# First expert tile: its x loaded early and its last rows added by matmuls; table and rank work moved behind it

## What is computed

```python
# 1 attention: full attention on inputs averaged over 4 tokens, repeated 4 times,
#   plus attention in a band |i-j| < 4 at full resolution
out_up = np.repeat(sm_attn(q_d, k_d, v_d), 4, axis=2)
scores = np.where(np.abs(pos[:, None] - pos[None, :]) < 4, scale * q @ k.T, -1e9)
x = out_up + softmax(scores) @ v                     # -> (2304, 512)
# 2 experts: 8 experts, each token goes to the best one only
logits = norm(x) @ norm(expert_emb).T / tau
expert_idx = np.argmax(logits, axis=1)
gate_w = softmax(logits)[arange, expert_idx]
out[mask] = gate_w[mask, None] * (relu(x[mask] @ w1[e]) @ w2[e])   # w1 512x1024, w2 1024x512
# 3 a dense layer: h = x @ w_in (512x2048); out = max(0.01*h, h) @ w_out
```

## Time and profile before

| | us |
|---|---|
| median of 3 runs | 922.05 |
| lowest and highest of them | 920.63, 927.44 |
| the profiled execution, its own time | 920.19 |
| span of the profile | 918.4 |
| TensorE busy in the span | 876.5 |
| VectorE, ScalarE, GpSimd busy | 537.9, 508.7, 177.3 |
| mean granted TensorE clock | 0.993 of full speed |

### The profile page before, as it was taken

How to read it: one execution, slowest core, us unless ns; L and a number is a source line. 1 busy time by engine, 2 the same in 40 slices (tenths; PEclk the granted TensorE clock), 3 DMA queues, 4 the chain that set the end, 5 groups by cost and what they waited for, 6 DMA issues and landing times.

```text
span 918.4 us, 17213 instructions
## 1 busy us (share of the span) xinstructions
PE 876.5 (95%) x5880; PEld 737.2 (80%) x5880; DVE 537.9 (59%) x797; ACT 508.7 (55%) x912; POOL 177.3 (19%) x259
## 2 busy tenths in 40 slices
PE   8898986899999999999998999999999999999997
PEld 4787765577777777787787998998898898898896
DVE  5677763789987888889987554224223223223222
ACT  3677775588887888888887443223223223223222
POOL 8666763014311101120001001101101101100000
PEclk9999998999999999999999999999999999999999
DMA  7586566418457627271101000100100100100000
GB/s 222 162 238 204 179 206 222 166 46 254 167 179 281 226 91 298 77 290 36 47 23 58 1 1 25 45 1 23 46 0 19 49 0 15 54 0 12 24 1 34
DMA packets 44844, 92.39 MB, mean 101 GB/s; under 512 B 4616, under 2 KB 23928, under 8 KB 40704
## 3 DMA queue, kind: packets, MB, share of 16 engines
q1 hardware_dynamic: 34928, 44.26, 15.9%
q0 software_dynamic: 9872, 47.53, 13.9%
HBM read 72.97 MB, written 18.81 MB: 100 GB/s over the span
## 4 chain that ended last, share of the span: by engine, by line
PE 80%; DVE 7%; issue 5%; ACT 5%; POOL 2%; another core or an unknown queue 0%; DVEq 0%; ACTq 0%; DMA 0%; SPq 0%; POOLq 0%
PE banks L872 69%; PE banks L807 2%; PE banks L904 2%; ACT ehi L1122 1%; DVE elo L1467 1%; PE banks L785 1%; DVE xTlo L1472 1%; PE banks L712 1%; PE banks L749 1%; PE banks L720 1%; PE banks L923 1%; ACT pdin L1025 1%; PE banks L761 1%; PE banks L779 1%; PE banks L879 1%
## 5 line engine op out<-in xcount | busy, mean ns | idle before, releaser
L1467 DVE TENSOR_TENSOR elo<-wslot,ehi 128x1024 fp32r<-128x1024 f32 x196 | 237.6, 1224 | 37.2 <-ACT ehi L1122 27.6
L1122 ACT ACTIVATE ehi<-wslot 128x1024 fp32r x196 | 204.9, 1059 | 44.6 <-PE banks L872 36.9
L1541 DVE SCALAR_TENSOR_TENSOR fg<-fraw 128x384 f32<-128x384 f32 x96 | 53.5, 557 | 212.5 <-ACT fraw L1209 203.0
L1209 ACT ACTIVATE fraw<-banks 128x384 f32<-128x384 f32 x96 | 47.2, 492 | 227.9 <-PE banks L872 226.9
L872 PE MATMUL banks<-zhi,winhi 128*128 (+1 forms) x384 | 130.5, 340 | 0.2 <-issue 0.2
L872 PE MATMUL banks<-zhi,winlo 128*128 (+1 forms) x384 | 129.4, 337 | 0.0
L872 PE MATMUL banks<-zlo,winhi 128*128 (+1 forms) x384 | 129.0, 336 | 0.0
L872 PE MATMUL banks<-wouthi,fhi 128*128 128x512 f32 x288 | 113.1, 393 | 3.4 <-DVE flo L1546 2.5
L872 PE MATMUL banks<-wouthi,flo 128*128 128x512 f32 x288 | 113.9, 395 | 0.0
L872 PE MATMUL banks<-woutlo,fhi 128*128 128x512 f32 x288 | 113.7, 395 | 0.0
L872 PE MATMUL banks<-ehi,xThi 128*128 128x512 f32 x200 | 83.1, 416 | 7.1 <-DVE xTlo L1472 7.1
(11 more groups left out here) (217 smaller groups left out, 1435.7 us busy)
## 6 DMA issues: line engine op xcount, KB each, us to landing
wslot<-in_w POOLq DMA_DIRECT2D x24, 1024.0 KB
wslot<-in_w SPq DMA_DIRECT2D x8, 1024.0 KB
xr<-xs SPq DMA_DIRECT2D x25, 272.0 KB
ys<-y_sb SPq DMA_DIRECT2D x25, 256.0 KB
qb<-in_qT SPq DMA_DIRECT2D x16, 288.0 KB, 4.0
kb<-in_kT SPq DMA_DIRECT2D x16, 288.0 KB, 4.9
vq<-in_vtok SPq DMA_DIRECT2D x32, 144.0 KB
vwin<-in_vtok SPq DMA_DIRECT2D x16, 245.0 KB
```

The costliest lines, as they stand in the source:

```text
L1122: act.activation(ehi[:, ring_at(k), :], wslot[:, chunk_cols(offs[dt], matrix, half, c)], ACT.Copy).then_inc(s_ehi, 1)
L1209: act.activation(fraw[:, f % 2, :], banks[:, f % 2, 0:TB], ACT.Copy).then_inc(s_fhev, 1)
L1467: dve.tensor_tensor(elo[:, ring_at(k), :], wslot[:, chunk_cols(offs[dt], matrix, half, c)], ehi[:, ring_at(k), :].bitcast(F32), ALU.subtra ...
L1541: dve.scalar_tensor_tensor(out=fg[:, f % 2, :], in0=fraw[:, f % 2, :], scalar=0.01, in1=fraw[:, f % 2, :], op0=ALU.mult, op1=ALU.max).then ...
```

## The change

Seven things, in the order of the program:

1. GpSimd clears `xs[0:128]` and the dummy rows at step 6 instead of the dummy rows alone ahead of step 0. Batch 0's scatter waits for that.
2. SyncE loads rows 0 to 127 of `xs` as soon as batches 0 to 2 are scattered, and GpSimd scatters batch 3 only after this load. The quarters of expert 1's weights are spread: the first goes ahead of the last `load_v`, the last behind tile 1's x.
3. VectorE makes `hot`, one 128x128 matrix of zeros and ones for each of batch 3's five tiles: a one where a token's `pos` is a row of tile 0. TensorE's `gather_x` multiplies batch 3's x by them and adds the early-loaded rows, which are turned by a multiplication with the identity, in the same PSUM bank: tile 0's x, turned. The `warm` matmuls change (12 and 5 instead of 4, 16, 12 and 16).
4. Tile 0's first weight chunks are rounded without the tables (expert 0 is always in the first half). The tables (`tables()`, with fewer steps) come after tile 0's x on VectorE; one step is folded into others (`skip`).
5. The gates' logits, the sorted ranks (two parts) and the gates' sums go behind tiles 1, 2, 3 and 4 on VectorE, the `Exp` on ScalarE into tile 2.
6. The loops over expert tiles are written out on TensorE, ScalarE, VectorE and SyncE; clearing of an expert's tail rows goes with the loads of x, one per tile.
7. GpSimd waits, for each expert from 2 on, until the first two quarters of its weights have landed before it issues the other two; the gates' scatters move from experts 2, 3, 4 to 5, 6, 7, behind the signal `s_w`.

```diff
@@ SyncE
+            load_quarter(1, 0)
             sp.wait_ge(s_o6, NPAIR - 3)
             load_v(NPAIR - 1)
-            for n in range(4):
-                if n:
-                    sp.wait_ge(s_wfirst[1], 16 * n)
-                load_quarter(1, n)
+            sp.wait_ge(s_wfirst[1], 16)
+            load_quarter(1, 1)
+            sp.wait_ge(s_zrow, 32)
+            for b in range(B - 1):
+                sp.wait_ge(s_scat[b], 16 * (TILES[b][1] - TILES[b][0]))
+            sp.wait_ge(s_o6, NPAIR)
+            sp.dma_start(xr[:, 0, :], xs[0:P, :]).then_inc(s_xl[0], 16)
+            sp.wait_ge(s_wfirst[1], 32)
+            load_quarter(1, 2)
...
             zero_rows(0)
-            sp.wait_ge(s_zero, 16)
-            for b in range(B):
-                sp.wait_ge(s_scat[b], 16 * (TILES[b][1] - TILES[b][0]))
-            sp.wait_ge(s_zrow, 16)
+            zero_rows(1)
+            sp.wait_ge(s_scat[B - 1], 16 * (TILES[B - 1][1] - TILES[B - 1][0]))
             sp.wait_ge(s_tab, 1)
-            sp.dma_start(xr[:, 0, :], xs[0:P, :]).then_inc(s_xl[0], 16)
-            for e in range(1, E):
-                zero_rows(e)
-            sp.wait_ge(s_zero, 16 * E)
-            load_x(1, 1)
...
+            for t in range(1, NT):
+                if t >= 2:
+                    sp.wait_ge(s_mx, t - 1)
+                if t < E:
+                    sp.wait_ge(s_zero, 16 * (t + 1))
+                load_x(t, t % 2)
+                if t + 1 < E:
+                    zero_rows(t + 1)
+                if t == 1:
+                    load_quarter(1, 3)
+                if t >= 3:
+                    store_y(t - 3)
@@ GpSimd
             for s in range(NSTEP):
+                if s == 6:
+                    gp.wait_ge(s_ready, 1)
+                    for at0 in (0, DUMMY):
+                        gp.dma_start(xs[at0:at0 + P, :], zrow[:]).then_inc(s_zrow, 16)
...
             indices(B - 1)
+            gp.wait_ge(s_xl[0], 16)
             scatter(B - 1, 0, MT)
...
                 for n in range(4):
+                    if n == 2:
+                        gp.wait_ge(s_wl[e % SLOTS], 64 * (e // SLOTS - 1) + 32)
@@ TensorE
-            warm(4, 3)
+            warm(12, 3)
             ranks(B - 1, NPAIR - 1)
-            warm(16, 3)
-            pe.wait_ge(s_tab, 1)
-            warm(12, 3)
-            pe.wait_ge(s_scat[B - 1], 16 * MT)
-            warm(16, 3)
+            warm(5, 3)
...
+            def gather_x():
+                pe.wait_ge(s_xr, 2 * NPAIR)
+                for j in range(MT):
+                    if j in (0, 2):
+                        pe.wait_ge(s_hot, 1 if j == 0 else 2)
+                    for c in range(KC):
+                        pe.matmul(banks[:, XB, c * P:(c + 1) * P], x_sb[:, (TILES[B - 1][0] + j) % SLOTX, c, 0:P],
+                                  hot[:, j, :], start=(j == 0 and c == 0), stop=False)
+                pe.wait_ge(s_xl[0], 16)
+                for c in range(KC):
+                    m = pe.matmul(banks[:, XB, c * P:(c + 1) * P], xr[:, 0, c * XC:c * XC + P], ident[:],
+                                  start=False, stop=(c == KC - 1))
+                m.then_inc(s_mx, 1)
...
-            turn_x(0, 0)
+            gather_x()
             hidden(0, 0, 0, 0)
-            with pe.Fori(0, NT - 2, 2) as t:
-                tile(t, 1, False)
-                tile(t + 1, 0, False)
+            for t in range(NT - 1):
+                tile(t, (t + 1) % 2, False)
@@ ScalarE
                 round_h(t, 0)
+                if t == 2:
+                    act.wait_ge(s_gate, 2)
+                    act.activation(gt2[:], gt2[:], ACT.Exp).then_inc(s_gate, 1)
...
+            for n, (matrix, _, half, c) in enumerate(FIRST):
+                act.activation(ehi[:, n, :], wslot[:, chunk_cols(0, matrix, half, c)], ACT.Copy).then_inc(s_ehi, 1)
+            sums_of_squares(B - 1, 0, MT)
+            round_chunks(0, range(0, HC), (0,))
             act.wait_ge(s_ss, NTOK)
             act.activation(gt1[:], ss_all[:], ACT.Sqrt).then_inc(s_gate, 1)
-            act.wait_ge(s_gate, 2)
-            act.activation(gt2[:], gt2[:], ACT.Exp).then_inc(s_gate, 1)
+            round_x(0)
+            relu(0, 0, chunk_no(0, 0))
+            round_chunks(0, range(HC, 2 * HC), (0,))
             act.wait_ge(s_tab, 1)
@@ VectorE
                 if b == B - 1:
+                    dve.wait_ge(s_pos, B)
+                    dve.wait_ge(s_slot_no, 1)
+                    for a, z in ((0, 2), (2, MT)):
+                        dve.tensor_tensor(hot[:, a:z, :], slot_no[:].unsqueeze(1).broadcast_to([NQ, z - a, P]),
+                                          pos[:, t0 + a:t0 + z].unsqueeze(2).broadcast_to([NQ, z - a, P]),
+                                          ALU.is_equal).then_inc(s_hot, 1)
...
                 rest_of_h(t, 1)
+                if t == 1:
+                    gate_logits()
+                if t == 2:
+                    rows_in_order()
+                if t == 3:
+                    places_in_order()
+                if t == 4:
+                    gate_sums()
                 rest_of_chunks(t + 1, range(0, 2 * HC), (off2,))
...
+            rest_of_chunks(0, range(0, 1), (0,))
             rest_of_x(0)
-            rest_of_chunks(0, range(0, 2 * HC), (off,))
+            tables()
+            rest_of_chunks(0, range(1, 2 * HC), (0,))
```

More of the change, by code:

```diff
@@ L231, in build @@
         cum = sb("cum", [P, E])
-        past = sb("past", [1, NT, E - 1])
-        past2 = sb("past2", [1, NT, E - 1])
+        past = sb("past", [1, NT, E])
+        past2 = sb("past2", [1, NT, E])
+        skip = sb("skip", [1, E])
         tl = sb("tl", [1, 4, NT])
@@ L1389, in _ @@
             dve.tensor_copy(zstart[:], run[0:1, :]).then_inc(s_zstart, 1)
-            link(dve.tensor_tensor(cnt[:], run[:], ebase[:], ALU.subtract))
-            sh = [P, E, N // P]
-            link(dve.tensor_tensor(over[:], row(cnt[:], sh, 2), row(thr[:], sh, 1), ALU.is_gt))
-            link(dve.tensor_reduce(ntile[:], over[:], AX, ALU.add))
-            link(dve.tensor_scalar(ntile[:], ntile[:], 1.0, None, ALU.max))
-            link(dve.tensor_tensor_scan(cum[:], ones_r[:], ntile[:], 0.0, ALU.mult, ALU.add))
@@ L1430, in _ @@
-            dve.tensor_scalar(pad[:, 2, :], ntile[:], float(P), float(-REG), ALU.mult, ALU.add)
-            dve.scalar_tensor_tensor(out=pad[:, 0, :], in0=ntile[:], scalar=float(P), in1=early[:],
-                                     op0=ALU.mult, op1=ALU.subtract)
-            link(dve.tensor_tensor_scan(sorted_end[:], ones_r[:], early[:], 0.0, ALU.mult, ALU.add))
-            sh, a = [NQ, NSORT, E - 1], slice(0, NSORT)
-            link(dve.tensor_tensor(reached[:, a], row(riota[:, a], sh, 2), row(sorted_end[0:NQ, 0:E - 1], sh, 1), ALU.is_ge))
```

180 lines of the change are left out of this document (95 added, 85 removed).

## The result

The changed kernel takes 915.23 us (median of 13 runs, 913.34 to 917.28), the kernel before on the same chip 920.63 (13 runs). The medians are 5.4 us apart, a ratio of 0.9941. Taken over all the runs of both kernels the ratio is 0.9924, with a 95% interval of 0.9908 to 0.9941: 0.6 to 0.8% faster, inside the band of 1% that I called no change, but clear of 1. The forecast was 913.0. The profiled execution took 915.58 us, with a span of 913.8: 4.6 less than the one before, where my sum had 8.5 less.

What follows compares the result with a forecast made beforehand. TensorE, 80% of the chain, was taken to bound the kernel, so only its waits count. Terms -8.2, -4.1, +1.4, +0.9, +1.5 sum to -8.5: 911.7 us from the profiled execution, 913.55 from the median; forecast 913.0, range 907.5 to 920.5.

Steps and rivals of the forecast that it cites:

- The stage change: Where attention hands over to the expert tiles: `project(0,0)` starts at 171.5 us instead of 179.74, -8.2 us.
- The half-width rows: Trace rows of f32 matmuls on half the array, about 0.11 us a record, giving 5.3 us for tile 0's gather.
- Loops: Expert tile loops written out: 0.37 us saved in each of 11 loop turns, -4.1 us.
- rival D: Written-out expert tiles: TensorE stops to fetch straight code, ten times at 2.0 us each, giving 933 us; chance 0.10.
- Rival C: Expert tiles fall to TensorE's own length, 12.4 us, 7.0 us more gained, giving 906 us; chance 0.15.
- VectorE's and ScalarE's work: Work put behind tiles 1 to 4: VectorE's pieces cost +1.4 us, ScalarE's `Exp` with its table load +0.9.
- Weights in two halves: At expert 4 only: the second half is issued after the first lands, costing +1.5 us, between 0 and 3.

Runs made afterwards that it cites:

- e7: Changed kernel with the first 20 matmuls of the gather done twice; 918.16 us beside 914.51 for the changed kernel on the same chip.
- e6: Kernel before with its tile loops written out, reloads of the weight offset kept; 919.50 us beside 921.44 for the kernel before.
- e3: Kernel before with its tile loops written out, without the reload of the weight offset; 910.83 us beside 914.75 for the kernel before.
- e1: Changed kernel with all four quarters of an expert's weights issued at once; 903.93 us beside 914.75 for the kernel before.
- e2: Kernel before with only the wait between the halves of an expert's weights added; 919.85 us beside 914.75 for the kernel before.
- e4: Changed kernel with VectorE's four pieces cut into eleven behind tiles 1 to 11, Exp in tile 9; 904.85 us beside 914.75 for the kernel before.
- e8: Changed kernel, quarters at once, last layer's weights after they land, VectorE's eleven pieces, Exp in tile 9, its table loaded early; 909.90 us beside 921.37 for the kernel before.

## Why the prediction was right in part, and which step failed

**The stage change: right.** `hidden(0,0)` started at 163.51 (163.35 foretold), the gather took 5.5 us (5.3), the tables were ready at 167.35 (167.4), x(1) was issued at 168.14 (168.4), `project(0,0)` started at 171.40 (171.5): -8.3 us against -8.2. The half-width rows were the right ones to size the gather by; the clock stayed at 1.00 through the 1.4 us of idle time. e7 shows that a slower gather has no slack, and the changed kernel's own chain shows ScalarE ready at 161.9 (162.0 foretold). The Trainium skill ("TensorE: Matmul & The Clock Gate", under "What overlaps and what doesn't", which stands in its section The mechanism) says that weight loads overlap running matmuls only where the row group differs. By that rule the gather would have taken 11.3 us; the trace disagrees for f32 at 128 columns too, with 5.5.

**Loops: right in kind, a little small.** -5.0 against -4.1. The long intervals lost 0.35 as foretold, and each short one a few hundredths more. I had put it on the branch and on the register that is loaded more; e6 rules the register out. Queue q8 has 39 packets of instructions after, 28 before, and no group of matmuls has a gap in it, so rival D did not come as I put it. The Trainium skill ("Runtime: NRT & Kernel Launch", section Instruction fetch mechanics) calls the fetching of straight code mostly hidden; the trace agrees for TensorE's own list. What may be left of rival D is at expert 4: in e3 its weights came 0.8 us later, with a packet of instructions in flight beside them, though no run tests that alone. Rival C did not come: 12.65, not 12.4.

**VectorE's and ScalarE's work: right.** +2.4 against +1.4 and +0.9, and piece by piece too. The interval with the Exp has +1.1 (0.9 foretold, and 0.2 for the logits), the next two, behind the sorted ranks, +0.6 and +0.7 (0.5 and 0.7), and the one behind the gates' sums nothing.

**"Weights in two halves": wrong.** The term was +1.5, between 0 and 3; the interval grew by 6.5, and ScalarE's wait was 6.7 us where I had foretold 3.5. I had priced the halves alone, by the start of one more DMA, and that ("a DMA's start and landing come twice") costs 2.3 us (e1) to 3.1 (e2) in the weights' time, at the top of the range. What the step left out is in e1, which has no halves and is still 3.8 us longer than the kernel before: 0.4 for the shorter tile, 2.0 for weights that come later (16.9 us and not 14.9), 1.6 for the clock (7.36 us for the 24 matmuls and not 5.8); that is 4.0 in sum, of which 0.2 did not reach TensorE. e3 and e6 show the same three without any other part of the change, 2.4 and 2.9 us. The sum took the loops as "11 x 0.37" and did not ask what a shorter tile, and more code to fetch, do to the one transfer that is awaited. And it weighed the clock at tile 0 only; here its fall costs 1.3 to 2.0 us for the next 24 matmuls (7.1 to 7.7 us and not 5.8; 2.7 in e4). With 6.5 for 1.5, the sum of 911.7 becomes 916.7, beside the 915.58 of the profiled execution; the rest is the loops (0.9 more than foretold) and the last layer (0.5), with 0.3 less won up to x(1).

So the mechanism of the gain was as foretold, and the gain was about half of what I had summed up: 4.6 us in the profiled execution for 8.5. That the time came out only 2.2 us above the forecast is in part luck. I had started from a median of 922.05 over 3 runs, where 13 runs give 920.63, and the stated range, 907.5 to 920.5, reached nearly to the kernel before itself. What makes one part of the weights late by 0.1 us in one run and by 2.4 in another is not shown.

## What to carry to other kernels

A transfer that ends one tile after its issue has a slack that every gain per tile eats: after each term that shortens a tile, or puts other traffic beside the transfer, sum again what is asked for one tile later. Price a wait on TensorE with the clock that it may lose, not by its length alone. Before splitting or reordering a load, ask what is read first and who is told: here a signal for the half that is needed was worth some 8 us, and the halves without it cost 5 by themselves in the kernel before.

## What the hardware showed unexpectedly

TensorE's granted clock fell after idle times that I had taken to be harmless: 1.48 and 1.02 us with four transposes between them (e3), 1.50 and 1.37 (e6), 0.64 and 1.02 (e8, where it fell 0.7 us into the next 24 matmuls, which took 7.34 us). It stayed at full rate after 0.28 and 1.18 (before) and after 1.41 (tile 0, changed kernel). The length of the wait alone does not decide: TensorE waits 1.72 to 1.76 us in the last expert tile in all 13 traces, and the clock fell behind it in one of them (e8, at 486.1 us).

A second half of a load, issued when the first has landed, leaves the DMA engines at 5% and then 53% of their time for about 4 us (282 to 286 in the changed kernel). The issue follows the landing by 0.3 us. Ahead of it only the last parts of the first half are still under way, one of them 1 us behind the others, and the second half's first part lands 4.6 us after its issue.
